# Moving scatters, filler products and weight loads in an attention and expert kernel for one core

## What is computed

```python
def reference(q, k, v, n_sink, window, w_gate, w1, w2, w_in, w_out):
    # attention: 4 batches, 8 heads of 64, 768 tokens, window 128, 4 sink tokens
    scores = q @ k.T / sqrt(64)              # kept where key < 4 or 0 <= query - key < 128
    a = softmax(where(keep, scores, -1e9))
    x = a @ v                                # (3072, 512)
    # experts: each token goes to the one of 8 with the largest logit
    e = argmax(x @ w_gate)
    y = gate * (relu(x @ w1[e]) @ w2[e])     # w1 (512, 1024), w2 (1024, 512)
    # last stage
    h = y @ w_in                             # (512, 2048)
    return (h - tanh(h)) @ w_out             # (2048, 512)
```

## Time and profile before

| what | value |
|---|---|
| median of 3 runs (lowest to highest) | 1085.21 us (1084.99 to 1085.94) |
| the profiled execution | 1091.07 us |
| its span, first to last instruction | 1089.3 us |
| busy: TensorE / VectorE / ScalarE / GpSimd | 98% / 61% / 44% / 46% |
| attention, experts, last stage | to about 180, 188 to 549, 549 to 1089 us |
| 60 to 100 us: TensorE / VectorE / ScalarE busy of 40 | 38.35 / 33.35 / 33.52 us |
| period of one expert slot | 12.28 us |
| ScalarE's split of one piece of weights | 0.97 us |

### The profile page before, as it was taken

How to read it: one execution, slowest core, us unless ns; L and a number is a source line. 1 busy time by engine, 2 the same in 40 slices (tenths; PEclk the granted TensorE clock), 3 DMA queues, 4 the chain that set the end, 5 groups by cost and what they waited for, 6 DMA issues and landing times.

```text
span 1089.3 us, 17071 instructions
## 1 busy us (share of the span) xinstructions
PE 1071.5 (98%) x5958; PEld 871.4 (80%) x5958; DVE 664.5 (61%) x1392; ACT 476.1 (44%) x1013; POOL 504.9 (46%) x521
## 2 busy tenths in 40 slices
PE   9999998999999999999999999999999999999997
PEld 6777775788888888888888888888888888888886
DVE  7888785634343444443378766666666666666664
ACT  7888883433242424442354433333333333333332
POOL 4385674706034527482274445335335335334433
PEclk9999998999999999999999999999999999999999
DMA  9556633616125344464231200101001011000001
GB/s 301 194 154 195 217 109 123 238 59 194 49 88 164 119 138 155 135 208 151 74 118 63 60 17 23 30 10 39 15 26 39 1 40 40 1 1 3 37 1 39
DMA packets 38204, 99.91 MB, mean 92 GB/s; under 512 B 8304, under 2 KB 8944, under 8 KB 33008
## 3 DMA queue, kind: packets, MB, share of 16 engines
q1 hardware_dynamic: 29248, 51.36, 15.2%
q0 software_dynamic: 8592, 47.31, 12.4%
q10 hardware_dynamic: 288, 0.26, 0.1%
HBM read 76.06 MB, written 22.86 MB: 91 GB/s over the span
## 4 chain that ended last, share of the span: by engine, by line
PE 89%; DVE 3%; issue 3%; POOL 3%; ACT 2%; DMA 1%; POOLq 0%; SPq 0%; DVEq 0%; ACTq 0%
PE bank L795 24%; PE bank L803 23%; PE bank L735 14%; PE bank L721 14%; PE bank L492 2%; PE bank L530 2%; PE bank L727 2%; PE bank L507 2%; PE bank L696 1%; PE bank L471 1%; POOL prob L1529 1%; ACT prob L872 1%; PE bank L779 1%; DVE xs L1306 1%; POOL sorted_x L1580 1%
## 5 line engine op out<-in xcount | busy, mean ns | idle before, releaser
L1559 POOL TENSOR_TENSOR weights<-raw,weights 128x1024 fp32r<-128x1024 f32 x70 | 166.7, 2402 | 195.1 <-ACT weights L864 194.1
L803 PE MATMUL bank<-weights,gT_hi 128*128 128x512 f32 x768 | 238.6, 392 | 0.3 <-DVE gT_lo L1426 0.3
L1662 POOL TENSOR_SCALAR ser<-ser 128x512 f32<-128x512 f32 x96 | 61.8, 644 | 280.8 <-DVE ser L1371 280.6
L795 PE MATMUL bank<-mT_hi,weights 128*128 128x512 f32 x768 | 189.8, 389 | 0.7 <-ACT mT_hi L1018 0.7
L795 PEld LDWEIGHTS bank<-mT_hi,weights 128*128 128x128 f32 x768 | 144.1, 188 | 30.8 <-ACT mT_hi L1018 0.9
L803 PEld LDWEIGHTS bank<-weights,gT_hi 128*128 128x128 f32 x768 | 142.6, 188 | 29.4 <-DVE gT_lo L1426 0.7
L803 PE MATMUL bank<-weights,gT_lo 128*128 128x512 f32 x384 | 149.6, 390 | 0.0
L735 PE MATMUL bank<-weights,hT_hi 128*128 128x512 f32 x464 | 148.7, 402 | 0.0
L1032 ACT ACTIVATE bank<-bank 128x512 f32<-128x512 f32 x96 | 55.9, 582 | 210.4 <-DVE ser L1402 210.4
L721 PE MATMUL bank<-weights,mT_hi 128*128 128x512 f32 x456 | 143.2, 395 | 0.0
L1664 POOL TENSOR_SCALAR sq<-sq 128x512 f32<-128x512 f32 x94 | 140.6, 1496 | 0.0
(11 more groups left out here) (163 smaller groups left out, 1594.5 us busy)
## 6 DMA issues: line engine op xcount, KB each, us to landing
raw<-w_all POOLq DMA_DIRECT2D x33, 1024.0 KB, 5.3
sorted_y<-ys SPq DMA_DIRECT2D x30, 261.0 KB, 3.1
xs<-sorted_x SPq DMA_DIRECT2D x29, 261.0 KB, 2.7
raw<-w_all SPq DMA_DIRECT2D x7, 1024.0 KB, 7.2
v_in<-vt SPq DMA_DIRECT2D x24, 256.0 KB, 3.8
kT<-kt SPq DMA_DIRECT2D x23, 264.0 KB, 3.2
qT<-qt SPq DMA_DIRECT2D x23, 256.0 KB, 4.0
raw<-sorted_y SPq DMA_DIRECT2D x20, 261.0 KB, 2.7
```

Source lines behind the costliest of these rows:

```text
L795: done = e.matmul(bank[HB[n % 3]][:, :], wt[:, f // 2, c, cols], x[:, c, :], start=(m == 0), stop=(m == 3 * CH - 1))
L803: done = e.matmul(bank[YB[i]][:, :], x[:, n % 3, rows], wt[:, f, :], start=(f == 0 and m == 0), stop=(f == GCH - 1 and m == 2))
L1559: e.tensor_tensor(lo, src, hi.bitcast(F32), ALU.subtract).then_inc(s_w_lo, 1)
L1662: e.tensor_scalar(row, row, SERIES_2, 1.0, ALU.mult, ALU.add).then_inc(s_ser, 1)
```

## The change

```diff
@@ tensor: turn of the last tile (i == ALL - 1), and the tail @@
                 if i == 0:
                     keep_warm(1, bank[O_BANK])
+                if i == ALL - 1:
+                    e.wait_ge(s_masked, H * ALL)
+                    keep_warm(2)
                 if not in_one_bank(i):
                     turn_prob(i, (1,))
 
             logits(ALL - 2)
             turn_prob(ALL - 1, (2,))
+            keep_warm(2)
             turn_prob(ALL - 1, (3,))
             keep_warm(2)
             turn_logits(ALL - 2)
             rank(MULTI - 1)
+            keep_warm(2)
 
             e.wait_ge(s_place, 2 * MULTI - 1)
@@ gpsimd: scatters_of and the loop over tiles @@
             def scatters_of(i):
                 for b, (start, tiles) in enumerate(SETS):
                     if tiles == TILES:
-                        each = 2 if b < 2 else 3
+
                         n = i - LAST[b] - 5
-                        if 0 <= n < tiles // each:
-                            yield from range(start + each * n, start + each * n + each)
+                        first = (0, 1, 2, 6) if b < 2 else (0, 3, 6, 6)
+                        if 0 <= n < 3:
+                            yield from range(start + first[n], start + first[n + 1])
                     elif i == LAST[b] + 4:
                         yield from range(start, start + tiles)
@@
                     if i < ALL and is_merged(i, p):
                         merge(i, p)
-                    if p != 1:
+                    if p == 1:
                         for g in to_scatter:
                             scatter(g)
                             break
@@ gpsimd: weight splits and loads of the expert stage @@
                 for j in range(4 if nxt < W_IN else 2):
                     split_lo(nxt, 2 * j)
+                    if nxt == 1 and j < 2:
+
+                        e.wait_ge(x_scaled, 2 + j)
                     if nxt == 1 and j == 0:
                         for late in range(len(RAW_AT), 4):
-
-                            e.wait_ge(x_loaded, 16)
                             e.wait_ge(s_w_lo, 2 * late + 2)
                             load_raw(1, late)
                     split_lo(nxt, 2 * j + 1)
                     e.wait_ge(s_w_lo, 8 * nxt + 2 * j + 2)
+                    if nxt == 1 and j == 0:
+                        continue
+                    if nxt == 1 and j == 1:
+                        load_raw(2, 0)
                     load_raw(nxt + 1, j)
```

## The result

The changed kernel takes 1080.23 us (median of 6 runs, 1079.77 to 1080.85), the kernel before 1085.1 us (6 runs, 1084.17 to 1085.94), both on one chip: a ratio of 0.9955 [0.9942, 0.9968], 4.9 us faster. The prediction had 1081.4, so 3.8 us, with a range down to 1078.6.

A forecast was written before the change was run, and what follows sets the result against it. TensorE, busy 98% of the span, was taken as the bound, so gains lay in its waits and half-clock stretch; -2.2 - 0.2 + 0.4 - 1.8 = -3.8 us from 1085.21 gave 1081.4 us, range 1078.6 to 1083.6.

The forecast's parts named there:

- The merges, -2.2: Attention tiles: with merge 1 directly behind merge 0, TensorE's four waits for merges go, -2.2 us.
- the 0.2 that I had for the sinks: Tiles 22 and 23: two of three scatters go behind the sink packing, -0.2 us.
- The doubtful step: Scatter between merges 1 and 2: merge 2 still starts in time, with 0.1 us to spare.
- The four scatters in tile 12, cost nothing: First batch's other four scatters land by 91.5, 2.3 us before VectorE's reciprocal of tile 12 needs them: no cost.
- rival (b): Merge gain partly taken by the next in line, or one slot wait stays: 1082.5, both 1083.5 us; chance 0.20.
- Products, +0.4: Last tile's three pairs of unread products overrun the pauses they fill, +0.4 us; no clock gain taken.
- Rival (a): Clock stays at its full level through the tail: 1078.5 us; chance 0.15.
- (c): Another engine was limiting and the waits reappear elsewhere whole: 1084.8 us; chance 0.06.
- (d): Slower: the low clock starts before the tail and lasts three times as long, 1088.2 us; chance 0.04.
- Slots, -1.8: Expert slots: GpSimd's splits and loads wait for VectorE's scalings; TensorE's 0.8 and 1.0 us waits go, -1.8 us.
- The pause: Tail: TensorE again idle some 2.7 us ahead of the last logits, then half clock for some 6.8 us.
- the bound of -2.9 us: Tail: most the unread products could give, if filling short pauses kept the clock at full level; not in the sum.

The follow-up runs named there:

- e5: Kernel before with only the scatters' places in a turn changed (one behind merge 1, the rest behind the guard), old counts: 1085.8 us against 1089.58, ratio 0.9966.
- e1: Kernel before, unchanged, profiled once more: 1085.02 us, ratio 1.0002; its profiled execution took 1086.54 us.
- e9: The changed kernel run again, no further edit: 1080.11 us, ratio 0.9961 against the kernel before.
- e2: Kernel before with both scatter edits alone (places and counts): 1081.93 us, ratio 0.9975.
- e11: The changed kernel run a third time, no further edit: 1084.96 us, ratio 0.995 against the kernel before.
- e10: Kernel before with new scatter places, old counts, and splits and loads waiting for the slots' scalings; no added products: 1079.02 us, ratio 0.9949.
- e6: Kernel before with only the scatter counts changed (1, 1, 4 and 3, 3), places as before: 1091.9 us, ratio 1.0021.
- e4: Kernel before with only the three pairs of unread products added, the first behind its wait for all masked scores: 1085.55 us, ratio 1.0007.
- e3: Kernel before with only GpSimd's waits for the second and third slot's scaling, late load and third expert's first two loads behind them: 1082.78 us, ratio 0.9983.
- e7: Kernel before with only the second and fourth split waiting for the scalings, loads issued as before: 1088.19 us, ratio 0.9991.
- set 1: Runs of the kernel before again and of each part alone, on one chip; the kernel before takes 1085.17 or 1085.02 us there.

## Why the prediction was right or wrong

**Direction and mechanism: right.** The change does what it says, waits go where it was forecast, and the time is in the range. The size was 3.8 us, and 4.9 was measured; three terms are behind that, and two of them err in opposite directions. The closeness of the total is in part luck. Two of the signs that the prediction named for being wrong were there: a wait for scatters at tile 14, and a full clock from 172 on.

**The merges, -2.2: mis-sized.** I priced the four waits by TensorE's idle time, 1.2 us for the first batch. From start to start the three tiles took 21.50 us and take 19.69, 1.8 less, and the second batch 1.6 less: 3.4 in place of 2.2. The step that failed is to take the idle column as the whole cost of a wait. Alone the place of the scatters brought 3.8 us in e5, with the 0.2 that I had for the sinks in it; its tiles 10 to 18 show 2.7 of that against e1. Of the rest, some can be the third slot, which was not held in e5's trace, though its edit does not touch the slots. The doubtful step held: the scatter between merges 1 and 2, with 0.1 us to spare, delayed nothing. The sinks' 0.2 us went too: e1 has a wait of 0.4 us for the sink packing of tile 22, the changed kernel none.

**The four scatters in tile 12, cost nothing: wrong.** The step that failed is the landing time: my slack of 2.3 us rested on 3.2 us, the median in a line for 24 scatters, where the trace has landings for the last three alone. The issue at 88.3 was right; the landing took 5.66 us. VectorE then waited 0.75 us in the changed kernel, 0.41 in e9, 0.45 in e2 and not at all in e11, and tiles 13 to 15 got slower by 0.76, 0.43, 0.47 and 0 us. With the old counts (e5, e10) these tiles take 20.23 us, as before, though landings are as long there: up to 4.9 us in e10's tiles 10 to 12 and 7.3 in its next batch. They are issued early enough. So the merges gave 1.2 us more than I had, and 0 to 0.8 of it was lost here; rival (b) had the form right, but the wrong place. The unequal counts are no gain: e6, with them alone, is slower, though the pauses of its set are in that number.

**Products, +0.4: not contradicted.** e4 measured +0.4, with an interval that includes none. In the changed kernel's traces only the second of the added pairs is on the chain: from the turns ahead of tile 22's logits to the placing of tiles 18 to 20 (L1194/L1199) the chain takes 2.94 us in the changed kernel and e9, and 2.69 and 2.70 in e2 and e10, which have no added products. Rival (a), the full clock, looks confirmed in the changed kernel's trace, with 1.00 from 172 on. It is refuted: e1 and e4 have the same clock with and without the products, and e11 has 0.50 with them. What went is the pause, and it had nothing to do with the change. Nothing speaks for rivals (c) and (d): no wait came back whole, and the mean granted clock of the changed kernel's profiled execution is 1.000.

**Slots, -1.8: mis-sized.** Both waits went, by the mechanism told: in e3, e7 and the changed kernel the scalings take 0.69 us. Against e1 they gave 2.4, not 1.8. The chains of e1 and after show the rest: each of the two waits was followed by a turn of 0.66 us where one without a wait takes 0.44, so 0.2 us came on top of each idle time, and the rest of 0.2 us I can't place. What the prediction didn't see is that the second wait hangs on when the rows land: the execution that it read, and e1, had it, and e2, e4 and e5 did not. Both its bounds ("only one goes", 0.8, and 1.9) took the wait as always there. "At 216.6 the fourth slot's scaling may be held" came true as 2.17 us at 204.94, and cost nothing.

**The pause: wrong.** I forecast a pause of some 2.7 us and 6.8 us at half clock in the changed kernel too. It wasn't there. A profiled execution 5.9 us over its own median, with one idle of 2.7 us and a low clock behind it, should have made me ask whether the timed runs have that pause at all. Since I gave it no part in the sum, the predicted time didn't suffer; the bound of -2.9 us and rival (a) were built on an idle that most timed runs of that set didn't have, by their 1085.

**What stays open.** The timed runs of the kernel before fall into two groups in set 1, most of them from 1083.4 to 1084.5 or from 1085.0 to 1085.9, while e10's lie within 0.16 us. The second slot wait, there or not, is a likely reason: it is worth 1.2 us, e4's profiled execution, without it, took 1084.11 us, and e1's, with it, 1086.54. It is not shown for the timed runs, which have no trace, and no run sets the landing on purpose. If it is the reason, the measured 4.9 us includes those 1.2, since the median of before lies in the slower group. Open too is what brings the pause.

## What to carry to other kernels

Price a removed wait by start to start of the unit that repeats, with the turn or product behind the wait in it, and not by the idle column alone. Keep GpSimd's long two-input work away from the moments when VectorE has an urgent operation with two SBUF inputs, and issue the last indirect scatter early where the reuse of a buffer waits for all of them: take its landing time from scatters of the same stage, and not from a median over the kernel. Where an operation squeezes through a gap of the other engine in one execution, look whether it does in the next. Before a feature of one trace enters the sum, see that its execution took the time of the timed runs.

## What the runs showed of the hardware

- A VectorE operation with two SBUF inputs beside GpSimd's split doesn't run slower in proportion. It takes 0.69 us alone and 1.76 to 5.78 us beside splits, and ends 0.54 to 0.57 us behind GpSimd's run of one or two splits. To start first does not help by itself: a start 0.40 to 0.47 us ahead of the split was held (before, e1, e6), one 0.52 or 0.53 us ahead was not (e2, e4, e5).
- An indirect scatter's landing varies within one kernel. In tiles 10 to 12 it took 2.9 to 5.1 us in e1, 3.3 to 4.9 in e10 and 3.0 to 5.3 in e9, whose longest is the fourth in one tile (5.66 in the changed kernel's first trace); in e10's second batch, two to a turn, 4.0 to 7.3.
- In some sets of runs ScalarE and VectorE saw TensorE's finished products some 2.5 us late, once or a few times in an execution, each time in a turn in which GpSimd issues scatters; a cause was not found. It cost some 5 us in 1085.
- The granted clock went with that pause: 0.50 behind it in the first execution of before and in e11, and 1.00 in e1 over 60 to 120, 150 to 190 and 186 to 215 us, through waits of up to 1.0 us. The Trainium skill ("TensorE: Matmul & The Clock Gate", section "HAM oscillation — how this bites in real kernels") has one long wait bring the clock down, and these rows agree, with TensorE's wait of 2.7 us. The next section there has many short pauses bring it down, and one place here is of that kind: in tile 18 of e6 TensorE stood three times, for 0.45, 0.26 and 0.17 us, and the clock was 0.57 over 132 to 136 us. In tile 12 of e6 it stood for 0.34, 0.40 and 0.24 us, and the clock stayed at 1.00.
